# Moving the expert weights' loads, the routing steps and the last mask to other engines and other rounds of an attention and experts kernel

## The reference

```
for t in range(S):
    state = alpha[:, :, t, :, None] * state + einsum('bhd,bhe->bhde', k[:, :, t], v[:, :, t])
    y[:, :, t] = einsum('bhd,bhde->bhe', q[:, :, t], state)
```

```
logits = (x / |x|) @ (emb / |emb|).T / tau
e = argmax(logits);  gate = softmax(logits)[e]
out = gate * (relu(x @ w1[e]) @ w2[e])          # w1: 384 x 1024, w2: 1024 x 384
```

## Time and profile before

| | |
|---|---|
| median of 3 runs | 939.15 us (937.91 to 939.63) |
| profiled execution | 939.15 us, span 937.6 us |
| PE busy | 888.5 us, 95% of the span |
| DVE / ScalarE / GpSimd busy | 441.7 / 321.8 / 272.9 us |
| attention | from the start to about 195 us |
| experts | about 200 to 513 us |
| output stage | from about 513 us to the end |

### The profile page before, as it was taken

One profiled execution on the slowest core, in us unless ns is written; L12 is line 12 of the kernel. 1 busy time (PEld: TensorE's weight loads), 2 busy tenths in 40 slices (PEclk: granted clock), 3 DMA queues, 4 the chain that ended last, 5 costly groups with the idle time before them and its releaser, 6 DMA issues. The chain is left out here.

```text
span 937.6 us, 16275 instructions
## 1 busy us (share of the span) xinstructions
PE 888.5 (95%) x5729; PEld 782.8 (83%) x5729; DVE 441.7 (47%) x830; ACT 321.8 (34%) x708; POOL 272.9 (29%) x281
## 2 busy tenths in 40 slices
PE   7999999777999999999998899999999999999994
PEld 4777877567999988999997789899999899999993
DVE  6788788663222222222223845445445445445442
ACT  2555656532222222222222223333323323323221
POOL 2213344631663476448721800100101001001001
PEclk8999999889999999999999999999999999999998
DMA  9787875538669677976822601001001001000000
GB/s 151 116 134 118 166 128 103 198 108 275 214 212 313 246 227 218 310 253 192 231 61 89 190 1 33 36 1 35 35 1 49 19 1 62 7 1 34 1 1 34
DMA packets 140975, 107.92 MB, mean 115 GB/s; under 512 B 103354, under 2 KB 129074, under 8 KB 140898
## 3 DMA queue, kind: packets, MB, share of 16 engines
q0 software_dynamic: 25696, 66.09, 21.8%
q1 hardware_dynamic: 115202, 40.79, 21.0%
HBM read 89.51 MB, written 17.35 MB: 114 GB/s over the span
## 5 line engine op out<-in xcount | busy, mean ns | idle before, releaser
L1148 PE MATMUL bank<-WX,hdTh 128*128 (+1 forms) x496 | 129.1, 342 | 4.5 <-DVE hdTl L1199 3.3
L1322 POOL DMA_INDIRECT out<-of,idi x24 | 23.6, 984 | 368.8 <-DVE of L1393 301.8
L1136 PE MATMUL bank<-WX,xdTh 128*128 (+1 forms) x372 | 118.9, 401 | 4.4 <-POOL WX L1080 2.5
L1080 POOL TENSOR_TENSOR WX<-raw_w,WX 128x3072 fp32r<-128x3072 f32 x14 | 95.3, 6825 | 79.5 <-DMA WX<-moe_w 67.4
L1366 PE MATMUL bank<-xT_h,wi_h 128*128 128x512 f32 x288 | 114.2, 396 | 0.1
L1366 PE MATMUL bank<-xT_l,wi_h 128*128 128x512 f32 x288 | 113.8, 395 | 0.0
L1366 PE MATMUL bank<-xT_h,wi_l 128*128 128x512 f32 x288 | 113.7, 395 | 0.0
L1433 DVE TENSOR_SCALAR em<-ee 128x512 f32<-128x512 f32 x96 | 50.6, 527 | 132.9 <-ACT ee L1411 130.6
L1411 ACT ACTIVATE ee<-bank 128x512 f32<-128x512 f32 x96 | 57.3, 596 | 146.3 <-PE bank L1366 146.3
L1414 ACT ACTIVATE g_h<-gg 128x512 fp32r<-128x512 f32 x96 | 60.7, 632 | 125.5 <-DVE gg L1438 120.5
L1442 DVE TENSOR_TENSOR g_l<-gg,g_h 128x512 fp32r<-128x512 f32 x96 | 70.5, 735 | 60.6 <-ACT g_h L1414 59.3
(11 more groups left out here) (205 smaller groups left out, 1412.0 us busy)
## 6 DMA issues: line engine op xcount, KB each, us to landing
WX<-moe_w POOLq DMA_DIRECT2D x14, 1536.0 KB, 15.9
raw_w<-moe_w POOLq DMA_DIRECT2D x14, 1536.0 KB, 11.1
xd<-sorted_x SPq DMA_DIRECT2D x31, 193.0 KB, 5.2
sorted_y<-yd SPq DMA_DIRECT2D x31, 192.5 KB, 4.1
xg<-sorted_y SPq DMA_DIRECT2D x6, 770.0 KB, 4.4
nat_a<-alpha SPq DMA_DIRECT2D x32, 144.0 KB, 3.2
nat_k<-k SPq DMA_DIRECT2D x32, 144.0 KB, 3.4
nat_q<-q SPq DMA_DIRECT2D x32, 144.0 KB, 3.6
```

What stands on the lines that cost most here:

```text
L1080: po.tensor_tensor(lower[:, cols], raw[x][:, :], upper[:, cols].bitcast(F32), ALU.subtract).then_inc(s_w, 1)
L1136: last = pe.matmul(bank[3 + i][:, :], xdT[t % 2][a][:, k * P:(k + 1) * P], WX[:, bass.ds(off + (b * WE + k * F + i * COLS), COLS)], start= ...
L1148: last = pe.matmul(bank[5][:, 0:DM], hdT[a][:, k * P:(k + 1) * P], WX[:, bass.ds(off + (b * WE + KD * F + k * DM), DM)], start=(k == 0 and ...
L1322: po.indirect_dma_start(out=out, out_offset=bass.IndirectOffsetOnAxis(ap=idi[:, GT * g + t:GT * g + t + 1], axis=0), in_=of[t][:, :], in_o ...
```

## The change

Seven things are moved or replaced:

1. In `SLOW` (batches 0 and 1), Ng and Nk stand after the scan F, and Ns, Nt, Nr in the round after.
2. The scatters of batches 0 and 1 are issued in rounds r = 4 and 5, no longer in 3 and 4.
3. The roots of batch 2 stand at the end of round 13 on GpSimd, behind the X steps and behind two new DMAs, U0 and U1: the upper parts of expert 0, now rounded by DMA. Wc, W2 and the halves are gone; DVE subtracts w1 and w2 (W0, W1) right after S5 in round 15.
4. The last pair has its C1 on ScalarE and its M1 on GpSimd, as every other pair.
5. The four loads of expert 1 (U0, U1 for the upper parts, V0, V1 for the raw ones) are issued on GpSimd at the end of round 15, before the roots of the last batch. The subtraction waits for the last scatter.
6. N0 comes after Ro, and both Xe steps of DVE after N0; the addition of its result is step P0 and the maximum P1. On ScalarE, Xe 0 goes ahead of SL, and Re0 of tile 0 stands behind Xe 1, ahead of Gq.
7. P0 is left out for the batches before the last, as P1 was before.

```
-                {"R": ("Rp", "Rr"), "S5": ("Ng", "Nk"), "LA": ("Ns", "Nt", "Nr")})
+                {"R": ("Rp", "Rr"), "F": ("Ng", "Nk")}, {"R": ("Ns", "Nt", "Nr")})
...
-        LAST = ({"LA": ("Rl", "Rx", "Dl", "N0", "Rc", "Rb", "Ro", "Rs", "Rn", "Rd", "Rw", "Rp", "Rr", "Rz", "Ng", "Nk", "Ns", "Nt", "Nr")},)
+        LAST = ({"LA": ("Rl", "Rx", "Dl", "Rc", "Rb", "Ro", "N0", "Rs", "Rn", "Rd", "Rw", "Rp", "Rr", "Rz", "Ng", "Nk", "Ns", "Nt", "Nr")},)
...
-            return [(name, n + lag) for name, lag in table if 0 <= n + lag < PAIRS
-                    and (name not in ("C1", "M1") or n + lag < PAIRS - 1)]
+            return [(name, n + lag) for name, lag in table if 0 <= n + lag < PAIRS]
...
             if n == PAIRS - 1:
                 i = place_of(out_, "S5") + 1
-                out_[i:i] = [("M1", n)]
-                out_ += [("W2", 0), ("W3", 0), ("NM", PARTIAL)]
-                out_.insert(place_of(out_, "M0") + 1, ("W1", 0))
-            if n == PAIRS - 2:
-                out_.append(("W0", 0))
+                out_[i:i] = [("W0", 0), ("W1", 0)]
+                out_.append(("NM", PARTIAL))
...
-                out_ += [("Wc", 0)] + [("SP", PARTIAL * C + j) for j in range(C)]
+                out_ += [("SP", PARTIAL * C + j) for j in range(C)]
...
                 elif b == PARTIAL - 1 and r == 1:
-                    i = place_of(out_, "M1")
-                    out_[i:i] = roots
-                    out_ += [(f"X{i}", b) for i in range(X_STEPS)]
+                    out_ += [(f"X{i}", b) for i in range(X_STEPS)] + [("U0", 0), ("U1", 0)] + roots
...
-                elif b < PARTIAL - 1 and r in (3, 4):
+                elif b < PARTIAL - 1 and r in (4, 5):
                     i = place_of(out_, "M1")
-                    out_[i:i] = [("SC", b * C + (r - 3) * HC + j) for j in range(HC)]
+                    out_[i:i] = [("SC", b * C + (r - 4) * HC + j) for j in range(HC)]
+            if n == PAIRS - 1:
+                out_ += [("U0", 1), ("U1", 1), ("V0", 1), ("V1", 1)]
...
+                    upper_, lower_ = (t[:, W12[i]] for t in parts_of(0))
+                    ve.wait_ge(s_raw0[i], 16)
+                    ve.wait_ge(s_hi0[i], 16)
+                    return ve.tensor_tensor(lower_, raw[i][:, :], upper_.bitcast(F32), ALU.subtract)
...
-                    if (name, p) == ("Ro", PARTIAL):
-                        d(("Xe", 0))
-                    if (name, p) == ("Rr", PARTIAL):
-                        d(("Xe", 1))
+                    if (name, p) == ("N0", PARTIAL):
+                        d(("Xe", 0), ("Xe", 1))
...
+                if name[0] == "U":
+                    if n:
+                        peA.wait(po, "Tq1", PAIRS - 1)
+                        veA.wait(po, "Qh1", PAIRS - 1)
+                    return upper_load(po, n, expert_at(po, n), int(name[1]))
+                if name[0] == "V":
+                    po.wait_ge(s_w, 2 * n - 1 + int(name[1]))
+                    return raw_load(po, expert_at(po, n), int(name[1]), s_raw)
...
-            e = expert_at(po, 1)
-            for x in range(2):
-                po.wait_ge(s_w, 1 + x)
-            po.wait_ge(s_xd[EARLY], 16)
-            po.wait_ge(s_xd[EARLY + 1], 16)
-            for x in range(2):
-                upper_load(po, 1, e, x)
-                raw_load(po, e, x, s_raw)
+            po.wait_ge(s_scat[PARTIAL], 16 * C)
```

50 lines of the change are left out of this document (20 added, 30 removed).

## The result

| | before | after |
|---|---|---|
| median | 937.98 us (933.38 to 940.61, 10 runs) | 946.09 us (940.63 to 950.61, 10 runs) |
| profiled execution | 939.15 us, span 937.6 | 951.5 us, span 949.9 |
| attention, KT0 of round 15 | 175.45 | 189.54 |
| first expert product | 200.07 | 212.37 |
| first product of the third tile | 225.28 | 241.46 |

What follows compares the result with a forecast made beforehand. It took PE to bound the kernel, so that outside one hollow every PE wait adds to the end. From 939.15 us the terms 1.5 + 3.4 + 2.8 - 5.4 + 3.3 - 0.6 - 2.2 - 0.7 gave 941.2 us, range 936.5 to 945.5.

Steps and rivals of the forecast that it cites:

- Part 8: Granted clock: falls to half behind two new waits, 1.5 us each, none at the one-hot; -0.7 us (-3.7 to +1.5).
- Part 2: Rounds 9 and 13: PE's YN1 waits for scatters issued one round later, 1.7 us each; +3.4 us.
- Part 6: Routing tail: N0 leaves the chain before the one-hot, -0.6 us; expert 1's earlier loads cost nothing (0 to +2).
- Part 1: Rounds 6 and 10: gate product behind scan F delays ScalarE's exponential; +1.5 us (0.5 to 2.5).
- Part 3: Rounds 13 and 14: roots behind new loads end the M1 wait but delay DVE's norm; +2.8 us (0 to 5).
- Part 4: Round 15: without ScalarE's copy of w1, PE's wait of 5.66 us shrinks to 0.3; -5.4 us (-5.7 to -4.5).
- Part 5: Last Yi1: GpSimd's M1 stands behind DVE's subtraction W0, so PE waits 4.0 us; +3.3 us net (0 to 6).
- Part 7: Experts: expert 1's earlier subtractions remove PE's wait at expert 5; -2.2 us (0 to -2.5).
- c: First expert tile: batch 2's scatters queue behind the two upper loads, tile 0 2 to 3 us late; 943.7 us, chance 0.10.
- Rival b: End of attention: W0 and W1 run without a gap and shut GpSimd out through both; 944.8 us, chance 0.12.
- a: PE's waits near 173 and 188: no longer than 2.15 us, so the clock holds; 935.6 us, faster, chance 0.17.
- d: Yi1 and scatters: M1 slips in at once, scatters land in 3.5 us; 939.4 us, no measurable change, chance 0.14.

Runs made afterwards that it cites:

- a_sc_early: The changed kernel with the scatters of batches 0 and 1 back in rounds r = 3 and 4: 943.57 us, ratio to before 1.0010.
- a_nk_early: The changed kernel with the gate steps (Ng, Nk, Ns, Nt, Nr) where the kernel before has them: 946.22 us, ratio to before 1.0089.
- after_again: The changed kernel itself, unedited, measured and profiled once more on another chip: 949.56 us, ratio to before 1.0072.
- a_roots_mid: The changed kernel with the roots of batch 2 between the X steps and the two loads of expert 0: 949.19 us, ratio to before 1.0076.
- a_roots_first: The changed kernel with the roots of batch 2 ahead of M1 in round 13 again: 946.98 us, ratio to before 1.0040.
- a_best1: The changed kernel with gate steps and scatters as before, and batch 2's roots between the X steps and expert 0's loads: 937.67 us, ratio to before 1.0006.
- a_best3: a_best1 with w2's upper part of expert 0 copied by DVE and only w1's loaded again: 932.47 us, ratio to before 0.9955.
- b_best: The kernel before with batch 2's roots behind the X steps and the early loads of expert 1: 932.18 us, ratio to before 0.9948.
- b_sc_late: The kernel before with only the scatters of batches 0 and 1 issued one round later: 942.72 us, ratio to before 1.0049.
- a_m1_on_dve: The changed kernel with the last pair's M1 back on DVE, ahead of W0 and W1: 956.75 us, ratio to before 1.0114.
- before_again: The kernel before with no edit, profiled on the chip of the fourth set: 937.62 us, ratio 0.9998.

## Why the prediction was wrong

The direction was right (0.51 on slower), the size was not: 2.1 forecast, 8.1 measured. The step that failed most is Part 8, the clock: -0.7 in the sum, where the profile has 7.7 us of longer products. With it failed the landing time in Part 2, and the start of the experts, which Part 6 took as unchanged.

Stage by stage, the profile against the terms of the sum: up to the start of round 15 it lost 14.1, forecast 9.2 (Parts 1 to 3 and the fall of 1.5 behind the wait near 173); from there to the first expert product it gained 1.8, forecast 4.9; the first two tiles lost 3.9, forecast nothing; the rest gained 3.9, forecast 2.2. Step by step:

- **Part 1** (+1.5): right in the changed kernel, +0.41 and +1.05. What I missed is that the part alone costs 1.9 more, since the scatters wait for the gate.
- **Part 2** (+3.4): the mechanism was right, the size failed. I took the landing of a scatter from round 12 (3.5 to 3.8 us). In the changed kernel's round 13 it was 4.82, and PE was idle 3.00 instead of 1.7; in its round 9 it was 3.35 and the idle there 0.30, but 1.13 came before it behind the late St1, and 1.9 of the 3.3 us lost are longer products at half clock. Alone, on a chip without the late St1, it was 5.05 in round 9 with an idle of 2.95, and the part cost 4.6 us. Undoing it took the changed kernel from 1.0072 to 1.0010. I had summed each round's wait alone, without a fall of the clock in round 9 or 13.
- **Part 3** (+2.8): the wait for M1 went and DVE idled before the norm, as forecast. PE's wait at YN1 in round 14 was 1.61 where I had 3.0, for PE came later itself. The two loads took more than I had: from the end of the last X step to the first root 2.2 us in the first profile and 3.5 in a_sc_early, for a forecast of 1.8; I had costed the gap ahead of a load at nothing, with 1.4 as its bound. Rounds 13 and 14 together lost 7.96 us: 3.5 of idle time, where Parts 2 and 3 gave 4.5, and 4.4 of longer products, where I had 1.5. So more than half of it is the clock. (By its own terms the time at which PE would be ready is 172.5 and not 172.3.)
- **Part 4** (-5.4): right as a local reading, the wait for `ktsb` is 0.60 instead of 5.66. Not all of it arrived: St1 of round 15 started 6.32 us after KT0, where in a_nk_early, on a chip without the late St1, it is 3.09, and PE was idle 1.97 before the next YN step.
- **Part 5** (+3.3): right in the first profile, 2.95 for a forecast of 4.0; in after_again, where PE came later itself, PE did not wait for the mask. The mask took 3.62 us beside a subtraction of 3.35 and 0.87 without one. The Trainium skill (GPSIMD Engine Reference, section Key points) says that GpSimd contends with VectorE instructions with two SBUF inputs, and these rows agree. With the mask back on DVE the kernel did not get faster.
- **Part 6** (-0.6, the rows at nothing): PE's idle before the one-hot was 1.67 instead of 3.01, but that the start of the experts keeps its length failed. I checked the rows of tile 2 for slack and not those of tile 0. The load of 3 MB more ahead of batch 2's scatters put the rows' load 8.55 us behind the last scatter instead of 4.80, and expert 1's loads behind made it land in 5.0 instead of 2.4: together they turned a slack of 6.3 us (rows' load of before issued at 186.66 and landed in 2.4, first transpose at 195.35) into 1.1. The changed kernel's own profile did not pay for it. The kernels with parts undone did: waits for the rows of 1.25 (a_roots_mid), 2.53 (a_nk_early) and 2.90 us (a_roots_first), and 10.50 in a_best1, which ate all of the 7.8 us saved before it. Half of the extra load taken away gave 0.5% (a_best3 against a_best1, on different chips). The 3.9 us of the first two tiles are the wait before the first M2 product and the half clock, and that wait goes with the chip.
- **Part 7** (-2.2): right, the wait at expert 5 is gone, also in b_best.
- **Part 8** (-0.7): wrong. The granted clock fell to half in rounds 9, 13 and 14 and from 199 to 216, behind idles of 1.13 (with 0.30), 3.00, 1.61 and 1.97 (with 2.95 and 1.67 to follow), and again at 226 behind 3.08. I had taken it that only idles of 2.15 to 3.01 and more count. The length of one idle does not settle it: 2.19 in round 13 of b_sc_late left the clock at 1.00. Five falls and not two, with mean clocks of 0.72 to 0.88 where I had costed two of 1.5 us. (For before, 6.3 us busy at half clock are 3.1 lost and not 2.5.)
- **The rivals**: c, the scatters behind the upper loads, which I gave 2 to 3 us and 0.10, did not come in the changed kernel, whose rows were 1.1 us early, but it is what held a_best1. The Trainium skill (DMA: Bandwidth & Descriptors, section SWDGE vs HWDGE vs iDMA) says that only one software queue is allocated; the row of q0 agrees. Whether the scatters waited for their turn in this queue or for their share of the 360 GB/s, no run tells apart: 1.5 MB at 360 GB/s is an estimated 4.2 us, and 4.3 were seen between a_best1 and a_best3. Rival b did not come: the mask ended at 201.77, between W0 and W1, and W1 took 0.67 us longer. Rivals a, d and e did not come either.

What stays open: why St1 and the first M2 product are late on two or three of the chips, how much of the 8.1 us is that (the changed kernel itself was never profiled on a chip without it; a_nk_early, which differs from it in the gate steps alone, lost 0.89% there), and the spread of a_m1_on_dve.

## What to carry to other kernels

Before a wait near the end of a stage is counted as a gain, look for the input of the next stage that comes by DMA, and write down when it was issued, when it landed and when it was first used: that slack is the most that any saving can bring. In a stage where PE is the limit, cost each new wait together with the slower products behind it: here they were more of the loss than the waits. Loading data a second time to spare an engine a copy costs the transfers queued behind it, here 11.4 us (a_best1) instead of 5.0 (before_again) from the last scatter to the next load. And two moves of a chain (a gate and the scatter that needs it) are to be costed as a pair: the late gate alone lost 0.93 us in each of two rounds, which it did not with the late scatters.

## What the runs showed of the hardware

- GpSimd's mask of 128x768 took 0.87 us alone and 3.62 beside a DVE subtraction of two SBUF tensors with 3072 columns, and ended 0.7 us behind it (201.77 and 201.04). The next subtraction had started at 200.95 and took 4.02 us instead of 3.35: GpSimd got its turn between two subtractions without a gap, and DVE stood for it.
- The landing of a scatter of 128 rows is no constant: the last one of round 9 was waited for until 3.35 us after its start in the changed kernel and 5.05 in b_sc_late, the last one of round 13 until 4.82 in one profile of the changed kernel and 2.80 in another, and batch 2's took 10.6 to 12.2 with 3 MB more of loads ahead (a_best1), 4.2 to 6.6 without (before_again).
- On some chips ScalarE started up to 2.3 us late (rounds up to 14) while GpSimd issued scatters, with the same instructions and all shown inputs ready; the kernel before took 942.6 and 943.4 us there and 937.2 to 937.6 on the others.
- The granted clock fell to half behind an idle of 1.61 us (round 14, changed kernel) and stayed at 1.00 behind one of 1.49 at the same place (a_best3) and behind one of 2.19 in round 13 of b_sc_late.
